# Order of the first weights' work around the end of a blocked attention: sums of x earlier or later, two loads and one weighing moved

## Time and profile before

| | us |
|---|---|
| median of 3 runs | 812.77 (811.79 to 813.98) |
| the profiled execution's own time | 813.94 |
| its span, first to last instruction | 811.2 |
| PE busy | 800.4 (99%) |
| DVE / ACT / POOL busy | 580.4 / 295.2 / 227.6 |
| mean granted TensorE clock | 0.998 of full speed |

### The profile page before, as it was taken

The page is one execution under the profiler, slowest core; times in us unless marked ns, Lnnn a source line. Parts: engine busy times, 40 slices in busy tenths (PEclk is TensorE's granted clock), DMA queues, the critical chain, the costliest instruction groups (busy, mean ns, idle before and its releaser), DMA issues.

```text
span 811.2 us, 11337 instructions
## 1 busy us (share of the span) xinstructions
PE 800.4 (99%) x4372; PEld 675.3 (83%) x4372; DVE 580.4 (72%) x960; ACT 295.2 (36%) x564; POOL 227.6 (28%) x231
## 2 busy tenths in 40 slices
PE   8989999999999999999999999999999999999998
PEld 7868888888888888888888888888888888888886
DVE  5977766766767767667657667677877777777766
ACT  4743222222222322322322322246544554545442
POOL 3976334333333433433433433242000000000000
PEclk9999999999999999999999999999999999999999
DMA  8931111120111121011111011010011101101004
GB/s 324 349 137 47 46 39 27 40 79 27 40 26 39 40 66 40 29 37 40 27 40 40 26 40 40 27 27 26 27 40 39 27 27 40 39 27 27 0 1 155
DMA packets 19864, 44.81 MB, mean 55 GB/s; under 512 B 2344, under 2 KB 2392, under 8 KB 19812
## 3 DMA queue, kind: packets, MB, share of 16 engines
q1 hardware_dynamic: 19812, 44.10, 17.2%
HBM read 40.93 MB, written 3.17 MB: 54 GB/s over the span
## 4 chain that ended last, share of the span: by engine, by line
PE 93%; DVE 2%; DMA 2%; POOL 1%; issue 1%; SPq 1%; ACT 1%; POOLq 0%
PE ps L1048 32%; PE ps L1029 28%; PE ps L1110 16%; PE ps L1129 16%; DMA att<-att_in 2%; DVE att L678 1%; POOL h_lo L452 1%; DVE w_lo L717 0%; SPq L287 0%; SPq L304 0%; ACT att L502 0%; DVE att L728 0%; DVE att L698 0%; DVE att L701 0%; DVE att L699 0%
## 5 line engine op out<-in xcount | busy, mean ns | idle before, releaser
L452 POOL TENSOR_TENSOR h_lo<-temps,h_hi 128x512 fp32r<-128x512 f32 (+1 forms) x128 | 134.9, 1055 | 298.5 <-ACT h_hi L566 298.5
L566 ACT ACTIVATE h_hi<-temps 128x512 fp32r<-128x512 f32 (+1 forms) x128 | 67.2, 525 | 338.3 <-DVE temps L794 338.3
L777 DVE TENSOR_TENSOR y<-ps,y 128x512 f32<-128x512 f32 x180 | 124.0, 689 | 71.7 <-PE ps L1048 71.7
L1029 PE MATMUL ps<-x_hi,w_hi 128*128 128x512 f32 (+1 forms) x448 | 151.0, 337 | 2.3 <-DVE temps L808 2.3
L1029 PE MATMUL ps<-x_lo,w_hi 128*128 128x512 f32 (+1 forms) x448 | 151.2, 338 | 0.0
L1029 PE MATMUL ps<-x_hi,w_lo 128*128 128x512 f32 (+1 forms) x448 | 151.2, 337 | 0.0
L1048 PE MATMUL ps<-h_hi,w_hi 128*128 128x512 f32 x384 | 150.5, 392 | 0.1
L1048 PE MATMUL ps<-h_lo,w_hi 128*128 128x512 f32 x384 | 150.3, 391 | 0.0
L1048 PE MATMUL ps<-h_hi,w_lo 128*128 128x512 f32 x384 | 149.4, 389 | 0.0
L1029 PEld LDWEIGHTS ps<-x_hi,w_hi 128*128 128x128 f32 x448 | 85.1, 190 | 15.0 <-DVE temps L808 2.7
L1029 PEld LDWEIGHTS ps<-x_lo,w_hi 128*128 128x128 f32 x448 | 85.0, 190 | 11.9
(11 more groups left out here) (83 smaller groups left out, 1110.1 us busy)
## 6 DMA issues: line engine op xcount, KB each, us to landing
w_raw<-w_in SPq DMA_DIRECT2D x96, 256.0 KB, 2.7
att<-att_in SPq DMA_DIRECT2D x24, 512.0 KB, 7.1
temps<-p_scr SPq DMA_DIRECT2D x4, 768.0 KB, 4.3
out<-y SPq DMA_DIRECT2D x12, 256.0 KB, 2.0
att<-dp_in SPq DMA_DIRECT2D x1, 24.0 KB
p_scr<-att SPq DMA_DIRECT2D x1, 24.0 KB
lam<-lam_in SPq DMA_DIRECT2D x1, 6.0 KB, 1.6
```

The source lines that it names most:

```text
L452: pool.tensor_tensor(hs_lo[side][:, f, at], ring(s, i), f32(hs_hi[side][:, f, at]), ALU.subtract).then_inc(s_hlo, 1)
L566: act.activation(hs_hi[s % SIDES][:, f, at], ring(s, i), ACT.Copy).then_inc(s_hhi, 1)
L777: dve.tensor_tensor(at, from_bank, at, ALU.add).then_inc(s_y, 1)
L1029: mm = pe.matmul(ps[:, bank, 0:CTS[side]], ww[q % 2][:, of], xx[side][:, 2 * x + k, :], start=(opens and k == 0 and n == 0), stop=(k == 1 ...
```

## The change

Five things are moved, and no arithmetic is added or removed.

1. SP: the loads of pieces 0 and 1 of quarter 0 are issued behind the two loads of unit 6 (the seventh), not ahead of them.
2. ACT: the high parts of both these pieces are made at p = 2; before, piece 0 at p = 1 and piece 1 at p = 2.
3. DVE: their low parts are made at p = 3 and p = 4, between the masks; before, at p = 2 and p = 3. `weigh` goes from p = 3 to p = 2.
4. DVE: at p = 5, `x_sums(4)` comes ahead of the low part of the weights' sums, `w1_piece(0, 2)`.
5. DVE: `x_sums(5)` comes behind U2 of step 0, not ahead of it.

```diff
@@ SyncE @@
             load_kv(5)
-            load_piece(0, 0)
-            load_piece(0, 1)
             for n in range(6, UNITS):
                 load_qk(n)
                 load_kv(n)
+                if n == 6:
+                    load_piece(0, 0)
+                    load_piece(0, 1)
@@ ScalarE @@
-                if 1 <= p <= 2:
-                    w1_piece(0, p - 1)
+                if p == 2:
+                    w1_piece(0, 0)
+                    w1_piece(0, 1)
@@ VectorE, loop over p @@
+                x_sums(p - 1)
                 if p == BLOCKS - 1:
                     w1_piece(0, 2)
-                x_sums(p - 1)
                 x_lows(p - 1)
                 if p + 1 < BLOCKS:
                     mask(2 * p + 2, (1,) if p == 1 else (0, 1))
...
-                    if 2 <= p <= 3:
-                        w1_piece(0, p - 2)
-                    if p == 3:
+                    if p == 2:
                         weigh()
+                    if p >= 3:
+                        w1_piece(0, p - 3)
                     mask(2 * p + 3)
-            x_sums(BLOCKS - 1)
-
@@ VectorE, step s @@
                 dve.tensor_tensor(v2, bank_b, p1, ALU.add).then_inc(s_u, 1)
                 if s == 0:
+                    x_sums(BLOCKS - 1)
                     x_lows(BLOCKS - 1)
```

## The result

The changed kernel takes 809.56 us (median of 12, 809.17 to 810.51), the kernel before 811.96 (median of 12, 811.0 to 813.98): a ratio of 0.997, 95% interval 0.9961 to 0.9978, so 2.4 us (0.3%) less. The forecast was 809.4, from 812.77. Of the two profiled executions the span fell from 811.2 to 807.6, by 3.6 where 3.5 had been worked out; the medians moved by less, and the experiments say why.

A forecast was written before the change was run, and what follows sets the result against it. PE alone bounds from `down(0, 0)` on. Wait 2.4 + clock 1.6 - PE's new wait for POOL 0.3 - locks 0.3 was given as about 3.5 us; from a median of 812.77, forecast 809.4, 8 in 10 within 808.0 to 811.2.

The forecast's parts named there:

- the wait at P7: Between P5 and P7, PE's idle time waiting for DVE's U2 was to go: 2.4 us won.
- The bound: From `down(0, 0)`, at 62.86 us, to the end PE alone bounds; an earlier start ends the kernel earlier by as much.
- a second thing that holds U2: In DVE's list the sums of pair 5 stand ahead of U2 and delay it, besides the late prod1.
- The margins behind U2: At P4 and P3, behind U2, PE was not to be held, by margins of 0.2 and 0.9 us.
- POOL as the new bound: At `down(0, 0)` PE, arriving at 58.7, was to wait for POOL's lows until 59.0 to 59.1; 0.3 us lost.
- its 0.4: At POOL's three `h_low` before `down(0, 0)`, 0.4 us added for DVE's `weighted` and POOL getting in each other's way.
- P1's start: P1 and all behind it were put 0.3 us later on balance, ends -0.5 and +0.8.
- the price of the locks: At p = 4, ahead of P1, DVE's two-operand low meets POOL's last sums of weights and q: 0.3 us lost.
- Moves 1 to 3 at nothing: Ahead of P1, DVE and ACT get earlier until the last masks, then about even; none of it reaches P1.
- The clock: In the 24 matmuls from P7, without the wait the clock stays at 1.00: 5.6 us, not 7.18; 1.6 won.
- rival A: Behind P5 the clock gives nothing, as a low stretch stays or typical executions had none: 810.7 us; chance 0.15.
- rival D: Pieces land late for POOL, and each us of waiting goes to P1: 814.8 us if 5.5 late; chance 0.03.

The follow-up runs named there:

- first: The kernel before, nothing moved, with GpSimd made to wait for the weights' low ahead of its low of pair 3: 809.57 us, 0.9968 of before.
- m123b: The kernel before with moves 1 to 3 alone, profiled a second time; it caught a long execution, span 809.7 us.
- m123c: The kernel before with moves 1 to 3 alone, profiled a third time; it caught a short execution, span 807.2 us.
- m4: The kernel before with move 4 alone: 808.82 us, 0.9963 of before.
- no5: The changed kernel without move 5, the sums of pair 5 back ahead of U2: 809.05 us.
- fill: The kernel before, order unchanged, with 10 extra matmuls between P5 and P7, results dropped: 811.07 us, ratio 0.999.
- m5: The kernel before with move 5 alone: 811.69 us, ratio 0.9994.
- m45: The kernel before with moves 4 and 5, without moves 1 to 3: 809.51 us.
- best: The kernel before with move 4, and the low of the second piece of w2 made by VectorE instead of GpSimd: 810.17 us.
- after2: The changed kernel again, unaltered: 809.45 us.
- m123: The kernel before with moves 1 to 3 alone: 809.18 us, 0.9972 of before; its first profile caught a long execution.
- late: The changed kernel with the two loads of weights issued one unit later, behind those of unit 8 (the eighth): 811.29 us.

## Why the prediction was right, and where it was not

In the two profiles the start of `down(0, 0)` moved by 3.68 us. Split at the places that the prediction used: P1 starts 0.24 earlier (0.3 later was forecast), the wait at P7 gave 2.44 (2.4), the 24 matmuls behind it 7.18 - 5.50 = 1.68 (1.6), and the stretch from step 1 to `down(0, 0)` took 0.66 more (0.3 more), 3.85 against 3.19. The terms as written add up to 3.4, not 3.5.

- *The bound.* Right: nothing behind `down(0, 0)` changed (741.13 of 741.14 us busy), and the span moved by 3.6.
- *Move 4.* Right: prod1 was forecast to end at 48.1 and ended at 47.9; the weights' low at 46.7 to 46.9, and ended at 46.4. The reading that it only waits for POOL is shown by first and by the pair m123b, m123c. By the exclusive lock that the Trainium skill states in "SBUF — State Buffer", section "SBUF: two separate sides", the one that comes second would end its own duration behind the end of the first. In m123b that is 43.23 + 2.35 + 1.22 = 46.80, measured 46.67; in m123c 42.97 + 1.23 + 2.37 = 46.57, measured 46.44. Rate sharing does not fit: the one that came first was not slowed.
- *Move 5.* U2 was forecast for 48.8 and ran at 48.76. But I named the sums of pair 5 as a second thing that holds U2, and they hold it only while prod1 is late: with move 4 in they end before U2's turn (m4, no5). Alone, move 5 takes 0.9 us off the wait at P7 and gains nothing that can be told; on top of move 4 it costs 0.4 us.
- *The margins behind U2.* 0.2 us at P4 held. I did not follow the chain to step 1: `weighted(0, 1)`, at 53.67, took 1.36 us against POOL, where it took 0.68 before, and `weighted(0, 2)` 1.07 (1.18 before). So `sum_of(0, 3)` was late, and P5 of step 1 started at 57.40, 0.64 behind its turn, 0.48 of it listed as idle.
- *POOL as the new bound.* Forecast: `down(0, 0)` held by POOL at 59.0 to 59.1; measured 59.18, after a stop of 0.25. But the stop is not new, it was 0.27 before (62.59 to 62.86, POOL's lows ending at 62.81). What is new in step 1 is the 0.64 at P5. The working also counts its 0.4 twice: three lows of 1.3 and 0.4 are 4.3, which gives 58.6. Measured, the three took 4.62 and started at 54.50.
- *P1's start.* The 0.24 us are scatter, not an effect of the change. The seven profiles whose lists are those of before up to what P1 waits for (before, fill, m5, m4, m45, first, best) have P1 at 45.05 to 45.81, the six with moves 1 to 3 and the loads as in the change (after, after2, no5, m123, m123b, m123c) at 45.53 to 45.83. In all of them P1 follows POOL's first sum of weights by nearly the same time: 19.4 us, and 19.5 where DVE's low at p = 4 comes ahead of POOL's decayed q (which then takes 2.78, not 2.52). So the price of the locks, put at 0.3, was 0.1. This chance of 0.24 and the unforeseen 0.64 at step 1's P5 nearly cancel.
- *Moves 1 to 3 at nothing.* The step that failed. They bring DVE to the weights' low 0.5 to 0.8 us earlier, level with POOL's low of pair 3, and in 10 of 14 executions, by their spans, that alone removes P7's wait. Inside the whole change it is worth nothing, as move 4 puts the sums there instead: after and after2 need 13.6 us from P1 to `down(0, 0)`, and so does m45 without moves 1 to 3. "None of it reaches P1" was right but for 0.1 us, but P7 was the thing to ask about.
- *The clock.* 1.6 forecast, 1.5 to 1.6 measured where it is there (7.18 or 7.20 against 5.62 or 5.64 behind the same wait; the 1.68 above has 0.1 more, as a first matmul that follows no wait is 0.1 shorter to the next start). It was in the profiled execution of before, and by span and clock in 36 of 62; the prediction counted it in full. Against the short group (about 809.2) the changed kernel (about 807.5) gains 1.7, against the long one (about 810.7) 3.2: a mean over executions of some 2.6, near the 2.4 measured. That is rival A in part. The forecast time came within 0.2 us of the measured one by luck: the gain was put 1.0 too high (3.4 against 2.4), and the 812.77 that it was taken from was 0.8 above the later median.
- *Move 1.* 0 was right, by a hair: m123b shows POOL waiting 0.48 us for the pieces, which landed at 26.4 as worked out. late shows rival D's mechanism and its price of one for one. In the changed kernel POOL starts them at 26.10 without a wait, so they had landed by then; no run shows why they came 0.3 later in m123b.

## What to carry to other kernels

When an instruction takes 2.4 times what its equals take, look at what the other engine began just before it: the place where the two meet may be worth more than the order of either list, and a wait that keeps them apart can be a gain. A wait of PE of about 2 us in a profile may cost a clock stretch too, but count it only where PE sets the pace behind the wait, and only in the share of executions that show it, so look at the clocks and spans of many. Compare intervals inside a trace (here from P1 to `down(0, 0)`), as the start of a stage can scatter by more than a small move is worth. Try each move alone: here one of five carried the gain, one cost, and three others would have done it in most executions, by an order decided within 0.1 us.

## What the runs showed of the hardware

- A VectorE instruction with two operands in SBUF and a GpSimd one wait for each other whole; the second ends 0.1 us before the first's end plus its own duration. 1.22 us became 3.42 or 2.88, 0.68 became 2.88, and GpSimd's 2.37 became 3.38. VectorE's sums with one operand in PSUM took 0.41 us beside them (after, 42.50, beside GpSimd's decayed q of 40.24) as without (before, 46.60, with GpSimd idle).
- Which goes first can change from run to run of one program: 42.97 against 43.06 (m123c), 43.25 against 43.23 (m123b).
- Behind a wait of 2.3 to 2.45 us the granted clock fell to the 1.2 GHz level in some executions (24 matmuls in 7.2 us) and not in others (5.62). By span and clock it fell in 36 of 62 executions of before, with PE kept busy in none of 11 (fill), and with a wait of 1.38 us in none of 11 (m5). In late it fell behind a wait of 1.84 us in the attention.
